# The combine before the gated layer: three steps move from VectorE to GpSimd and ScalarE

## The reference

```python
# 1: linear attention with a forget gate, per head
state = f[t][:, None] * state + outer(k[t], v[t]);  y[t] = q[t] @ state
# 2: mixture of 8 experts, the 2 best per token, shares from a softmax over the two
out[token] += share * (relu(x @ w1[e]) @ w2[e])
# 3: RMS norm and a gated layer of width 1536
rms = sqrt(mean(x * x) + 1e-6);  xn = x / rms * rms_g
g = xn @ w_gate;  result = (g * sigmoid(g) * (xn @ w_val)) @ w_out
```

## Time and profile before

| | us |
|---|---|
| median of 3 runs | 1240.45 (1239.44 to 1245.13) |
| the profiled execution's own time | 1240.45 |
| its span, first to last instruction | 1238.8 |
| PE busy | 1190.9 |
| DVE busy | 690.6 |
| ACT busy | 476.0 |
| POOL busy | 481.3 |

### The profile page before, as it was taken

One profiled execution on the slowest core, in us unless ns is written; L12 is line 12 of the kernel. 1 busy time (PEld: TensorE's weight loads), 2 busy tenths in 40 slices (PEclk: granted clock), 3 DMA queues, 4 the chain that ended last, 5 costly groups with the idle time before them and its releaser, 6 DMA issues.

```text
span 1238.8 us, 25021 instructions
## 1 busy us (share of the span) xinstructions
PE 1190.9 (96%) x8085; PEld 1041.2 (84%) x8086; DVE 690.6 (56%) x1216; ACT 476.0 (38%) x963; POOL 481.3 (39%) x463
## 2 busy tenths in 40 slices
PE   4999999999989999999999998999999999999997
PEld 4777787778879999999999898888888888888886
DVE  7888888886534454544444455445445454454433
ACT  3666656555334343333433333332322323223211
POOL 8468787764653517163367552220020201100000
PEclk9999999999999999999999999899999999999999
DMA  6233333353567868687788864130030301101000
GB/s 226 72 109 121 128 131 107 101 177 148 174 191 231 243 211 253 199 259 223 235 254 257 252 211 138 52 103 26 26 77 26 102 26 53 50 26 52 26 1 26
DMA packets 109091, 164.78 MB, mean 133 GB/s; under 512 B 48336, under 2 KB 84944, under 8 KB 108496
## 3 DMA queue, kind: packets, MB, share of 16 engines
q1 hardware_dynamic: 97296, 115.68, 30.0%
q0 software_dynamic: 11712, 47.98, 12.4%
HBM read 107.45 MB, written 56.16 MB: 132 GB/s over the span
## 4 chain that ended last, share of the span: by engine, by line
PE 80%; POOL 6%; DVE 4%; issue 4%; DMA 3%; ACT 2%; SPq 0%; DVEq 0%; POOLq 0%; ACTq 0%
PE pD L1962 16%; PE pD L2061 12%; PE pA L2061 12%; PE pA L1991 9%; PE pS L1991 8%; PE pA L2075 6%; PE pA L1773 5%; PE pX L2075 3%; PE pS L2075 3%; POOL qk L698 1%; DVE W L1257 1%; POOL fT L679 1%; POOL prods L714 1%; DMA stage<-w 1%; POOL qk L697 1%
## 5 line engine op out<-in xcount | busy, mean ns | idle before, releaser
L1962 PE MATMUL pD<-we,xsH 128*128 x612 | 189.5, 391 | 0.0
L1773 PE MATMUL pA<-W 64*128 64x128 f32 (+3 forms) x1920 | 137.3, 284 | 15.2 <-DVE W L1257 12.2
L1706 DVE TENSOR_TENSOR gs<-pD,sig 128x512 f32<-128x512 f32 x72 | 49.8, 692 | 174.8 <-ACT sig L1191 174.8
L1773 PEld LDWEIGHTS pA<-W 64*128 64x128 f32 (+3 forms) x1920 | 113.2, 171 | 34.4 <-DVE W L1257 18.0
L918 POOL DMA_INDIRECT pair<-y_sorted,y_row x40 | 39.7, 994 | 252.6 <-DMA z_rows<-pair 231.6
L1962 PEld LDWEIGHTS pD<-we,xsH 128*128 128x128 f32 x612 | 114.1, 188 | 22.1 <-issue 0.2
L1962 PE MATMUL pD<-we,xsL 128*128 x306 | 120.0, 392 | 0.0
L1991 PE MATMUL pA<-we,hidH 128*128 (+1 forms) x464 | 118.6, 336 | 1.0 <-issue 1.0
L1191 ACT ACTIVATE sig<-pD 128x512 f32<-128x512 f32 x72 | 43.2, 600 | 198.1 <-PE pA L2061 198.1
L1437 DVE STREAM_TRANSPOSE pA<-hidP 128x512 f32<-128x512 f32 x98 | 64.7, 705 | 92.9 <-DMA hidP<-hid_rows 92.6
L1257 DVE TENSOR_TENSOR W<-W,prods 128x512 f32<-128x512 f32 (+1 forms) x120 | 101.8, 855 | 23.3 <-PE pA L1773 21.3
(11 more groups left out here) (281 smaller groups left out, 2695.1 us busy)
## 6 DMA issues: line engine op xcount, KB each, us to landing
hid_rows<-hid SPq DMA_DIRECT2D x49, 512.0 KB, 3.2
hidP<-hid_rows SPq DMA_DIRECT2D x196, 128.0 KB, 2.9
stage<-w POOLq DMA_DIRECT2D x48, 384.0 KB, 4.6
qk<-qk_t SPq DMA_DIRECT2D x24, 512.0 KB, 3.7
y_sorted<-yo SPq DMA_DIRECT2D x55, 192.0 KB
xs<-x_sorted SPq DMA_DIRECT2D x200, 48.0 KB, 2.0
fT<-f_t SPq DMA_DIRECT2D x12, 512.0 KB, 4.0
vN<-v_n SPq DMA_DIRECT2D x24, 256.0 KB, 2.7
```

Of the source, the lines that this page charges most:

```text
L1706: dve.tensor_tensor(gs[:], pD[:, f % 2 * 512:f % 2 * 512 + TT], sig[f % 2][:], ALU.mult).then_inc(s_u, 1)
L1773: ins = pe.matmul(pA[par][keys, s, c * P:(c + 1) * P], both[r, 1, c, keys], both[r, 0, c], start=True, stop=True)
L1962: ins = pe.matmul(hidden_bank(t, h), (xsL if a else xsH)[t.par][:, k * P:(k + 1) * P], we[:, bass.ds(at + (b * WE + k * F + h * HF), HF)], ...
```

## The change

The multiply, multiply and add of the combine run on GpSimd (three instructions where VectorE had two), between the gathers. Only two `second` buffers are left, so the second gather of group j+2 is issued behind the combine of group j, which also needs a wait of GpSimd on its own add. The wait on `s_tx` goes, since `xs0` and `xs1` are no longer written. Square and row sum become one ScalarE activation with an accumulator per j, followed by a square root of one column; the first of them waits for `FIRST * TS` on `s_first`, which is the add of the last group. VectorE takes a reciprocal per j and scales the group.

```diff
--- before.py
+++ after.py
@@ -295,7 +295,7 @@
         xs += [sb(f"xs{i}", [P, DM]) for i in (2, 3)]
         where[0] = first_at
         z_first = sb("z_first", [P, TS, DM])
-        second = [sb(f"second{i}", [P, DM], at=in_region_at + 4 * DM * i) for i in range(2)] + xs[0:2]
+        second = [sb(f"second{i}", [P, DM], at=in_region_at + 4 * DM * i) for i in range(2)]
         assert slot_i_at >= in_region_at + 8 * DM
         xsH = [sb(f"xsH{i}", [P, DM], F32R) for i in range(2)]
         xsL = [sb(f"xsL{i}", [P, DM], F32R) for i in range(2)]
@@ -900,13 +900,28 @@
                     out=to, out_offset=None, in_=y_sorted[:, :],
                     in_offset=bass.IndirectOffsetOnAxis(ap=y_row[:, j, k:k + 1], axis=0)).then_inc(s_pair[j], 16)
 
+            def combine_first(j):
+
+                own, other = z_first[:, j], second[j % 2][:]
+                pool.wait_ge(s_pair[j], 32)
+                pool.tensor_scalar(own, own, share[:, j, 0:1], None, ALU.mult).then_inc(s_first, 1)
+                pool.tensor_scalar(other, other, share[:, j, 1:2], None, ALU.mult).then_inc(s_first, 1)
+                pool.wait_ge(s_first, FIRST * j + 2)
+                pool.tensor_tensor(own, own, other, ALU.add).then_inc(s_first, 1)
+
             pool.wait_ge(s_yrow, 10)
             stored = pool.value_load(rows_stored_i[0:1, 0:1], min_val=16, max_val=16 * SLOTS)
             wait_alone(pool, s_ys, stored)
-            pool.wait_ge(s_tx, SLOTS)
-            for j in range(TS):
+            for j in range(2):
                 take_first(j, 0, z_first[:, j])
                 take_first(j, 1, second[j][:])
+            for j in range(TS):
+                if j + 2 < TS:
+                    take_first(j + 2, 0, z_first[:, j + 2])
+                combine_first(j)
+                if j + 2 < TS:
+                    pool.wait_ge(s_first, FIRST * (j + 1))
+                    take_first(j + 2, 1, second[j % 2][:])
 
             pool.wait_ge(s_ys, 16 * SLOTS)
             pool.wait_ge(s_tz, KC)
@@ -1196,8 +1211,15 @@
                     act.wait_ge(s_o, t.times(F2C, f - 1))
                 act.copy(uH[f % 2][:], u[f % 2][:]).then_inc(s_uh, 1)
 
-            act.wait_ge(s_rms, TS)
-            act.activation(rms_first[:], ms_first[:], ACT.Sqrt, scale=1.0 / DM, bias=eps[:]).then_inc(s_rms, 1)
+            for j in range(TS):
+                act.wait_ge(s_first, FIRST * TS)
+                if j >= 2:
+                    act.wait_ge(s_rms, 2 * j - 3)
+                act.activation(second[j % 2][:], z_first[:, j], ACT.Square,
+                               accum_out=ms_first[:, j:j + 1]).then_inc(s_rms, 1)
+                act.wait_ge(s_rms, 2 * j + 1)
+                act.activation(rms_first[:, j:j + 1], ms_first[:, j:j + 1], ACT.Sqrt, scale=1.0 / DM,
+                               bias=eps[:]).then_inc(s_rms, 1)
             for k in range(KC):
                 high_z(Tile(0, None, 2), k)
             act.preload_act_table_set("sigmoid_and_others")
@@ -1654,19 +1676,6 @@
             slots(dve, slot)
 
 
-            def combine_first(j):
-
-                own, other = z_first[:, j], second[j][:]
-                dve.wait_ge(s_pair[j], 32)
-                dve.tensor_scalar(own, own, share[:, j, 0:1], None, ALU.mult).then_inc(s_first, 1)
-                dve.wait_ge(s_first, FIRST * j + 1)
-                dve.scalar_tensor_tensor(out=own, in0=other, scalar=share[:, j, 1:2], in1=own, op0=ALU.mult,
-                                         op1=ALU.add).then_inc(s_first, 1)
-                dve.wait_ge(s_first, FIRST * j + 2)
-                dve.tensor_tensor(other, own, own, ALU.mult).then_inc(s_first, 1)
-                dve.wait_ge(s_first, FIRST * j + 3)
-                dve.tensor_reduce(ms_first[:, j:j + 1], other, AX.X, ALU.add).then_inc(s_rms, 1)
-
             def combine(t, j):
 
                 dve.wait_ge(s_pair[j], t.times(32, 32))
@@ -1719,11 +1728,9 @@
                     dve.tensor_copy(fin[t.par][:, j], out_bank(j)).then_inc(s_fin, 1)
 
             for j in range(TS):
-                combine_first(j)
-            dve.wait_ge(s_rms, TS + 1)
-            dve.reciprocal(inv_first[:], rms_first[:]).then_inc(s_normed, 1)
-            dve.wait_ge(s_normed, 1)
-            for j in range(TS):
+                dve.wait_ge(s_rms, 2 * j + 2)
+                dve.reciprocal(inv_first[:, j:j + 1], rms_first[:, j:j + 1]).then_inc(s_normed, 1)
+                dve.wait_ge(s_normed, 2 * j + 1)
                 dve.tensor_scalar(z_first[:, j], z_first[:, j], inv_first[:, j:j + 1], None,
                                   ALU.mult).then_inc(s_normed, 1)
             for k in range(KC):
@@ -2079,7 +2086,7 @@
 
             pe.wait_ge(s_last, 2 * THIRDS)
             for j in range(TS):
-                pe.wait_ge(s_normed, j + 2)
+                pe.wait_ge(s_normed, 2 * j + 2)
                 for k in range(KC):
                     ins = pe.transpose(first_bank(k)[:, j * P:(j + 1) * P], chunk(z_first[:, j], k), ident[:])
                     if j == TS - 1:
```

## The result

| | before | after |
|---|---|---|
| median, us | 1240.59 (1239.44 to 1245.13, 4 runs) | 1253.74 (1251.81 to 1257.19, 4 runs) |
| ratio | | 1.0088, 95% interval 1.006 to 1.0115 |
| profiled execution's span, us | 1238.8 | 1253.7 |
| last matmul of the slots ends | 769.18 | 774.30 |
| first gather of wide tile 0 | 755.95 | 761.20 |

The change makes the kernel slower, by 0.9% (0.6 to 1.15%), which is 10.9 us on the 1240.45 of the prediction. The direction was forecast, the size not quite: 8.1 us were forecast.

What follows compares the result with a forecast made beforehand. PE bounds the kernel, with an uncovered gap before stage 3. Terms -0 (wait), +6.6 (combines), +3.4 (ScalarE), -1.9 (VectorE and PE to high_z) sum to +8.1 us on 1240.45: 1248.6 us, range 1243.5 to 1252.5.

Steps and rivals of the forecast that it cites:

- The path: Hand-over from last slot to stage 3: PE's uncovered 3.66 us gap, so the change's effect is the shift of high_z.
- The rival by which GpSimd's part hides (C): Hand-over: GpSimd's combines hide under PE's last slots, not slower; needs 1.1 us per combine; chance 0.04.
- The rival of a cheap multiplication (A): GpSimd's combine: multiplications at the cast's rate, 0.42 us each; shift +2.8 to +5.1, time 1243.2 to 1245.6; chance 0.22.
- rival B: GpSimd's stream: multiplications cost 1.45 us (+11.1, 1251.5 us), or the last gather lands late; chance 0.12.
- the late landing: Group 3's last gather, before its combine: landing after 5.25 us would add up to 1.1 us; forecast counted 0.
- the dearer multiplication: GpSimd's combine: 1.45 us per multiplication at the strided product's rate, making the stream 3.0 us longer.
- the forecast's 1.08: GpSimd's combine: one 128x384 multiplication takes 1.08 us, from the TENSOR_SCALAR row's 2.75 ns per column.
- first gather to last add: GpSimd's gathers and four combines before wide tile 0: from 755.95 to 778.30, 22.35 us.
- squares and roots: ScalarE behind the last add: four squares with roots, all uncovered, 778.32 to 782.05; 3.75 us in the table.
- last root to `high_z`: Last group's reciprocal and scaling on VectorE, then PE's transpose, until high_z: 1.32 us where 3.22 stood before.
- slow start of PE, change: First matmuls of stage 3 after the gap: the lower clock's cost of 2.4 us stays the same, change 0.
- I carry the 2.4 over unchanged: PE's start of stage 3: a longer gap cannot lower the clock further, so its 2.4 us cost stays.

Runs made afterwards that it cites:

- one multiplication less: Changed kernel without GpSimd's second multiplication per combine (output changes): first gather to high_z 24.11 us, ratio to the kernel before 1.0043.
- kernel with the constant: Changed kernel with both shares in GpSimd's multiplications replaced by 0.5: first gather to high_z 28.40 us, single execution 1252.60 us.
- before again: Kernel before, unedited, profiled a second time: first gather to high_z 19.10 us, ratio 0.9996.
- ScalarE's part alone: Kernel before with per-group squares and roots on ScalarE behind VectorE's last combine, four buffers kept: first gather to high_z 19.22 us, ratio 1.0005.
- squares behind their group: Changed kernel with each ScalarE square waiting for its own group's add, not the last: first gather to high_z 26.71 us, ratio to the kernel before 1.0064.
- two buffers, VectorE: Changed kernel with its two buffers and interleaved gathers, but VectorE's two-instruction combine: first gather to high_z 19.64 us, ratio 1.0017.
- repeated share: Changed kernel with each GpSimd multiplication written as a two-tensor product, share repeated along the row: first gather to high_z 25.36 us, single execution 1247.64 us.
- the version meant to beat both: Kernel before with VectorE summing groups 0 and 1, ScalarE squaring groups 2 and 3, earlier roots and scaling: first gather to high_z 17.72 us, ratio 0.999.
- GpSimd's combine alone: Changed kernel with squares, sums, root and scaling put back as before: first gather to high_z 29.86 us, ratio 1.0082.
- all gathers first: Changed kernel with four second buffers and all eight gathers ahead of the four combines: first gather to high_z 28.74 us, ratio 1.0082.

## Why the prediction was right, and where its size was off

The path was read rightly. The gap before wide tile 0 has no cover, everything in it is serial, and the distance after `high_z` does not change. The rival by which GpSimd's part hides (C) needed a combine in 1.1 us; it takes 3.5. The rival of a cheap multiplication (A) fell by its own row: 1.25 us, 3.3 ns per column, where the cast has 0.97. VectorE takes 0.41 for it. The Trainium skill, GPSIMD Engine Reference, section Engine selection, has one-input work roughly at line rate, and no TENSOR_SCALAR row here agrees. Its factor of about 2 for two-input work is nearer: the add takes 0.99 us, VectorE's square of the same shape 0.56.

Of rival B, the late landing is refuted (one multiplication less took its full 4.9 us off), and the dearer multiplication is half true: it lies between the forecast's 1.08 and B's 1.45.

From the first gather, `high_z` came 29.01 us later where the prediction had 27.42. Step by step:

| step | predicted | measured |
|---|---|---|
| first gather to last add | 22.35 | 24.32 |
| of it 8 multiplications | 8.64 | 9.9 |
| of it 4 adds with their waits | 4.0 | 4.3 |
| of it 2 gathers behind a wait on the add | 0.15 idle each | 0.28 and 0.27 idle |
| squares and roots | 3.75 | 3.46 |
| last root to `high_z` | 1.32 | 1.23 |
| slow start of PE, change | 0 | -0.07 |

The term that was mis-sized is the multiplication. The prediction scaled the 128x1024 row by columns, 1.06 to 1.08. The kernel with the constant took 1.18 for 384 columns where the 1024 of the earlier trace rows take 2.82. If the operator does not matter, which no run shows, a line through the two is about 0.2 us fixed and 2.6 ns per column. A proportion leaves the fixed part out, and it weighs more at 384 columns than at 1024. The column of shares adds 0.07. The prediction gave the add a little fixed time and the multiplication almost none. It had no second row of this instruction, but its own show a two-tensor operation of 16 columns at 0.22 us, where 2.29 ns per column would give 0.04.

GpSimd's stream was forecast 2.0 us too short: 1.3 of it are the multiplications, 0.3 the adds, and 0.4 the starts of gathers and combines. ScalarE gave back 0.3, as each square starts 0.2 us into the root before it and not behind it (786.39 after 786.19), and the way to `high_z` 0.1. That leaves the 1.6.

The forecast of 8.1 thus becomes 9.7 us by the profile's local distance, and the ratio says 10.9 with an interval of 7.4 to 14.3, which holds both. The absolute time of 1248.6 was further off than the difference. The median of four runs, 1253.74, lies above the stated range, which ended at 1252.5; the median of all 19, 1252.32, lies just inside, and the ratio on the starting 1240.45 gives 1251.4. The prediction took three runs of the kernel before for its level and allowed nothing for their spread, and they lay some 3.5 us below the level that the longer series found.

The step "I carry the 2.4 over unchanged" held for this pair by luck and is no rule, as the last section shows. One reading is a little off: a granted clock of 0.75 over 781 to 782 puts the rise at 781.5, and not at 781.25.

## What to carry to other kernels

Work moved from a faster to a slower engine is free only under cover. In this hand-over nothing covered it, its whole extra duration was lost, and the idle share of the engine that took it (POOL was busy for 39%) said nothing. Where the price of an instruction is scaled from a larger shape, fixed time has to be added, and the range should hold it. Two profiles of one kernel can differ by microseconds ahead of the edit, so compare distances between marks around it, not spans.

## What the runs showed of the hardware

PE's slow start after the gap is not one number. The first 18 matmuls of stage 3 take 4.20 us at the full clock. In the twelve profiles they took 6.61 (before), 6.13 (before again), 6.54 (after), 6.10 (ScalarE's part alone), 6.83 (squares behind their group), 7.27 (one multiplication less), 7.24 (two buffers, VectorE), 6.06 (constant), 7.17 (repeated share), 6.36 (the version meant to beat both), and only 4.46 with GpSimd's combine alone and 4.47 with all gathers first. In the last two PE was idle for 14.25 and 12.43 us, in the changed kernel for 12.98, and in the kernel with the constant for 12.42; so the length of the gap does not decide. The `high_z` of the last two is 461.4 us from the end instead of 463.5. The windows of PE (us, busy, granted clock, DMA share, GB/s) in the kernel with GpSimd's combine alone:

```profile
790.00:791.00 1.00, 0.98 (x5) 0.50 0.00 0
791.00:792.00 1.00, 0.00 (x0) 0.78 0.00 0
792.00:793.00 1.00, 0.88 (x4) 1.00 0.00 0
```

and in the changed kernel:

```profile
794.00:796.00 2.00, 2.00 (x6) 0.50 0.52 126
796.00:797.00 1.00, 1.00 (x5) 0.83 0.52 169
```

In the first the clock rises from its lower level, 1.2 GHz, to 2.4 GHz in an idle microsecond behind twelve transposes without a pause, before the first matmul of stage 3 at 792.12. In the second the transposes came in four groups with pauses, and it rises 4.6 us after the matmuls began (791.74). A closed row of transposes is not needed for the early rise: with all gathers first they come in four groups too, and the clock is back at 0.90 in the microsecond from 788, where the first matmul of stage 3 starts at 789.36. What decides is open. Over the twelve profiles the slow start costs 0.3 to 3.1 us. Whether the executions of one kernel spread as far is not shown; the two of the kernel before differ by 0.5.

The fall is no more regular: the clock dropped to its lower level some 2 us after PE's last matmul in the kernel before, and about 5 us after it in the changed kernel, by this window:

```profile
778.00:780.00 2.00, 0.00 (x0) 0.82 0.35 97
```
